# Second token mixing of a fused mixer network: the order of token splits, middle-layer splits and residuals on the vector and scalar engines

## The reference, cut to what matters

```python
def _moe2_ref(x, w_tok1, w_tok2, w_ch1, w_ch2):
    xt = x.transpose(0, 2, 1)
    h = np.maximum(xt @ w_tok1, 0.0) @ w_tok2      # 576 tokens -> 256 -> 576 tokens
    u = x + h.transpose(0, 2, 1)
    h2 = np.maximum(u @ w_ch1, 0.0) @ w_ch2        # 512 channels -> 1536 -> 512
    return (u + h2).astype(np.float32)
```

## Time and profile before

| | |
|---|---|
| time, median of 3 runs | 1283.67 us (1279.82 to 1286.72) |
| time of the profiled execution | 1284.21 us |
| its span in the profile | 1282.4 us |
| PE busy | 1206.6 us (94% of the span) |
| DVE busy | 820.4 us (64%) |
| ACT busy | 502.9 us (39%) |
| POOL busy | 368.4 us (29%) |
| granted TensorE clock, mean | 0.973 |

### The profile page before, as it was taken

How to read it: one execution, slowest core, us unless ns; L and a number is a source line. 1 busy time by engine, 2 the same in 40 slices (tenths; PEclk the granted TensorE clock), 3 DMA queues, 4 the chain that set the end, 5 groups by cost and what they waited for, 6 DMA issues and landing times.

```text
span 1282.4 us, 20593 instructions
## 1 busy us (share of the span) xinstructions
PE 1206.6 (94%) x7590; PEld 1168.7 (91%) x7590; DVE 820.4 (64%) x1220; ACT 502.9 (39%) x796; POOL 368.4 (29%) x216
## 2 busy tenths in 40 slices
PE   5989999999999999988687999999999899999998
PEld 5889999999898999887576899999999899999998
DVE  3776776676767676755353547667666775666664
ACT  3533334252425243423312245555555543333331
POOL 3443425344444424320641122322221420000000
PEclk9999999999999999989888999999999999999999
DMA  9824444352717230508737487867659999999982
GB/s 254 160 44 100 75 106 78 87 97 53 131 37 145 39 74 0 151 4 254 251 128 271 157 295 261 275 245 267 228 222 313 343 358 274 258 278 269 278 207 50
DMA packets 348428, 228.12 MB, mean 178 GB/s; under 512 B 268880, under 2 KB 316368, under 8 KB 347344
## 3 DMA queue, kind: packets, MB, share of 16 engines
q1 hardware_dynamic: 348368, 227.32, 61.6%
HBM read 136.84 MB, written 92.80 MB: 179 GB/s over the span
## 4 chain that ended last, share of the span: by engine, by line
PE 59%; issue 13%; DVE 10%; DMA 8%; POOL 4%; SPq 3%; ACT 2%; DVEq 0%; POOLq 0%; ACTq 0%
PE bank L42 11%; PE bank L43 10%; PE bank L44 10%; PE bank L1193 8%; PE bank L1194 8%; PE bank L1195 8%; DMA qkv_x_tokens<-x_tokens_scratch 3%; PE bank L252 2%; DVE weights_fraction L621 1%; SPq L154 1%; POOL z_z L797 1%; DVE tokens_cos L618 1%; DMA weights_down<-w_scratch 1%; DMA tokens_down<-w_scratch 1%; DVE attention_u L1094 1%
## 5 line engine op out<-in xcount | busy, mean ns | idle before, releaser
L42 PE MATMUL bank<-weights_tok,z_z 128*128 128x288 f32 x576 | 175.5, 305 | 14.7 <-ACT z_z L471 9.2
L43 PE MATMUL bank<-weights_tok,z_z 128*128 128x288 f32 x576 | 171.3, 297 | 0.0
L44 PE MATMUL bank<-weights_tok,z_z 128*128 128x288 f32 x576 | 171.2, 297 | 0.0
L42 PEld LDWEIGHTS bank<-weights_tok,z_z 128*128 128x128 f32 x576 | 109.8, 191 | 18.2 <-ACT z_z L471 10.6
L43 PEld LDWEIGHTS bank<-weights_tok,z_z 128*128 128x128 f32 x576 | 109.8, 191 | 0.0
L44 PEld LDWEIGHTS bank<-weights_tok,z_z 128*128 128x128 f32 x576 | 109.6, 190 | 0.0
L782 POOL TENSOR_TENSOR weights_rms_inverse<-weights_mean_squares,weights_minus_half 128x8 f32<-128x8 f32 x40 | 65.5, 1637 | 139.2 <-DVE weights_mean_squares L588 139.1
L797 POOL TENSOR_TENSOR z_z<-tokens_cos,z_z 128x512 fp32r<-128x512 f32 x32 | 51.3, 1604 | 178.9 <-ACT z_z L471 178.1
L478 ACT ACTIVATE weights_x_channel_major<-attention_u 128x288 fp32r<-128x288 f32 x64 | 28.4, 444 | 151.5 <-DVE attention_u L650 151.5
L42 PE MATMUL bank<-weights_x_channel_major,weights_ch 128*128 128x288 f32 x256 | 77.2, 301 | 0.0
L43 PE MATMUL bank<-weights_x_channel_major,weights_ch 128*128 128x288 f32 x256 | 75.4, 294 | 0.0
(11 more groups left out here) (272 smaller groups left out, 3750.8 us busy)
## 6 DMA issues: line engine op xcount, KB each, us to landing
g_scratch<-attention_staged SPq DMA_DIRECT2D x36, 960.0 KB, 4.6
weights_g<-g_scratch SPq DMA_DIRECT2D x24, 1152.0 KB, 8.3
g_scratch<-attention_staged SPq DMA_DIRECT2D x36, 384.0 KB, 4.7
x_scratch<-attention_u SPq DMA_DIRECT2D x8, 1152.0 KB, 4.5
u_scratch<-attention_u SPq DMA_DIRECT2D x8, 1152.0 KB, 9.9
weights_raw_u<-u_scratch SPq DMA_DIRECT2D x6, 1536.0 KB, 8.2
qkv_u_left<-u_scratch SPq DMA_DIRECT2D x12, 768.0 KB, 9.7
qkv_k<-in_k_dram SPq DMA_DIRECT2D x32, 256.0 KB, 5.0
```

Of the source, the lines that this page charges most:

```text
L42: eng.matmul(out, w[0], x[0], start=first, stop=False)
L43: eng.matmul(out, w[0], x[1], start=False, stop=False)
L44: return eng.matmul(out, w[1], x[0], start=False, stop=last)
```

## The change

Two orders are changed, and no instruction is added or taken away.

- ACT, for each batch: before, the first token piece of the next batch, then both halves of the middle layer, then the other token pieces. After: the middle layer's first half, the first token piece, the middle layer's second half, then the other token pieces.
- DVE, for each batch: before, both low parts of the middle layer, then the three token pieces of the next batch ahead of residuals 0, 2 and 4. After: first low part, first token piece, second low part, the other two token pieces, and then all eight residuals.

```diff
@@ phase_b, scalar
         def batch(n):
+            hidden_hi(n, 0)
             if n + 1 < B:
                 x_hi(act, n + 1, 0)
-            for mt in range(NM):
-                hidden_hi(n, mt)
+            hidden_hi(n, 1)
             for piece in range(1, NPX):
                 if n + 1 < B:
                     x_hi(act, n + 1, piece)
@@ phase_b, vector
         def batch(n, i, pair, more=True):
-            for mt in range(NM):
-                hidden_lo(n, mt)
+            hidden_lo(n, 0)
+            if more:
+                x_lo(dve, n + 1, 0)
+            hidden_lo(n, 1)
+            for piece in range(1, NPX):
+                if more:
+                    x_lo(dve, n + 1, piece)
             for g in range(NG):
-                if more and g % 2 == 0 and g // 2 < NPX:
-                    x_lo(dve, n + 1, g // 2)
                 residual(n, i, pair, g)
                 if isinstance(pair, int) and (n, g) in PREP_LO:
                     nxt["prep_lo"](dve, 0, PREP_LO[n, g])
```

## The result

The changed kernel takes 1254.28 us (median of 4 runs, 1252.93 to 1255.22) against 1283.75 (median of 4 runs) for the kernel before: a ratio of 0.9771 with a 95% interval of 0.9743 to 0.9799. The forecast was 1253. A second set of five runs gave 1252.43 us (0.9762, 0.974 to 0.9783). The profiled execution took 1252.93 us with a span of 1251.1.

The account below looks back on a forecast made before the run. PE was taken to stall because the middle layer queued on ACT behind the next token load. Gains of 33.7 us less losses of 2.9 gave 30.8, so 1284.2 became 1253.4, forecast 1253; own range 1249 to 1259, overall 1248 to 1270.

Parts of the forecast that it names:

- The cycle and its bound: Middle layer of batch n queues on ACT behind batch n + 1's token load; bound by PE, a batch takes 12.8 us.
- Part 1, ACT's order: On ACT, the first middle-layer half no longer waits for the token load; weight step done by E + 3.6.
- Part 2, DVE's order: On DVE, second low part by E + 1.65, 0.75 us before PE needs it; token pieces done by E + 3.4.
- E: The end of hidden(n), the hidden matmuls of batch n on PE; the forecast's times count from it.
- Part 3, what moves with it: SP issues the token load at E + 3.4, with nearly 2 us of room; the store just fits before residual 0.
- The sum: Over PE's mixes: 23.2 us of stalls plus 9.8 of half clock, 33.0; with batch 1's 0.7, 33.7 us.
- Batch 1: PE's mt 1 begins at 621.1, idling 4.9 us instead of 5.61, clock low as before: +0.7 us gain.
- (a): In batch 1 POOL may get in ahead of DVE's small token piece, delaying group 6; bounds 0 and 1.5, 0.7 us taken.
- (b): Batches 5 and 6: late store 4 and line 1249's load delay residuals; bounds 0 and 5, 2.2 us taken.
- POOL's lock in every batch: Rival, 0.08: POOL wins over DVE's small token piece in batches 1 to 4, costing 16 us in all: 1268.
- Load still late: Rival, 0.17: token load takes 9.6 us, cycle 14.3 us, PE idle between mt 0 and mt 1: 1270, or 1261.

Follow-up runs that it names:

- the half clock alone: Kernel before, with 32 extra matmuls of 288 columns on PE filling the stall ahead of each mix of batches 1 to 6: 1280.18 us (0.9973).
- the pieces in a row: Kernel before, with all three token pieces on DVE behind both low parts and ahead of residual 0, ACT as before: 1271.4 us (0.9894).
- one residual ahead: Changed kernel, with residual 0 of each batch moved ahead of the second and third token pieces on DVE: 1278.52 us (0.9962).
- with POOL only writing: Pieces in a row, with POOL's channel-weight work replaced by clearing, so it reads nothing and output is not the reference's: 1255.18 us (0.9781).

## Why the prediction was right

*The cycle and its bound.* Right. The load's wait is gone, and a batch bound by PE takes 12.75 us where 12.8 was worked out. The clock is 1.00 in batches 2 to 4, and ACT's wait for the load fell from 72.0 to 4.3 us.

*Part 1, ACT's order.* I described it as what frees the middle layer. It does so mainly in batch 1, where the first half of the mix runs during the wait. In the others the load is there in time, and the old order costs little: PE waits 0.81 us for ACT in batch 3, and the time is 1256.08 us against 1254.28, which the intervals do not tell apart. That the two parts are not alike in weight the prediction did not say.

*Part 2, DVE's order.* The times were right (the last piece done at E + 3.8 instead of 3.4, second low part well before it is needed). What was not seen is that the old order tied the load to the store, by way of residual 0, and to POOL. The prediction gave DVE's order the load's earlier issue; it did not say that ACT's order alone would fail, and the expectation for that run missed by 9 us for the same reason.

*Part 3, what moves with it.* Right, and narrowly: residual 0 waits 0.28, 0.18 and 0.70 us for the store in three batches, the load lands before it is wanted, and with its issue 4.3 to 6.0 us later nearly the whole gain is lost.

*The sum.* 33.7 us for stalls and half clock, of which 29.5 were measured between batch 1 and batch 7, after the losses. As a count of what PE would no longer lose it held. As two separate gains it did not: the half clock alone, mended in four batches, gave 0.4 us from batch 1 to 7. That the time came within 1 us of the forecast is in part luck: the two profiled executions of the changed kernel took 87.5 and 90.8 us from batch 1 to 7, with 0.2 us between their times.

*Batch 1.* Forecast +0.7 less 0.7 for POOL, measured -0.2. PE idles 4.77 us in the middle of the mix and then 1.48 ahead of group 6, which is (a) at its upper bound: POOL, which had asked meanwhile, got in between two DVE pieces. The rows of the changed kernel, DVE and POOL:

```profile
617.56 2.24 DVE L1068 TENSOR_TENSOR tokens_x_token_major<-qkv_x_tokens,tokens_x_token_major 128x1024 fp32r<-128x1024 f32 x1 [4.64 <-ACT tokens_x_token_major L1019]
...
621.57 3.85 DVE L1071 TENSOR_TENSOR tokens_x_token_major<-qkv_x_tokens,tokens_x_token_major 64x512 fp32r<-64x512 f32 x1
```

```profile
620.93 3.94 POOL L1145 TENSOR_TENSOR weights_up<-weights_raw_up,weights_up 128x1536 fp32r<-128x1536 f32 x1 [2.21 <-ACT weights_up L1040]
```

*The loss (b) in batches 5 and 6.* The size was near by luck (2.2 forecast, 2.6 + 0.3 measured), as the cause was wrong. In batch 5 residual 0 did not wait for store 4, and the load of line 1249 held DVE for 0.1 us at most. ACT stood still before the small token piece, the small low piece and residual 0 behind it, and PE behind that (ACT, DVE and PE of the changed kernel):

```profile
677.64 0.63 ACT L1019 ACTIVATE tokens_x_token_major<-qkv_x_tokens 128x512 fp32r<-128x512 f32 x1 [3.56 <-issue]
```

```profile
678.30 0.69 DVE L1071 TENSOR_TENSOR tokens_x_token_major<-qkv_x_tokens,tokens_x_token_major 64x512 fp32r<-64x512 f32 x1 [2.96 <-ACT tokens_x_token_major L1019]
```

```profile
679.53 0.40 PE L42 MATMUL bank<-qkv_tok,z_hidden_tok 128*128 128x288 f32 x1 [2.31 <-DVE attention_u L1094]
```

ACT waited for nothing that the profile shows; before, the same instruction had 1.98 us of this, hidden. ACT stands still ahead of this one instruction in every profile taken here, for 1.98 to 3.75 us. In both kernels it falls in a stretch with the DMA engines full (share 1.03 and 1.04), and instruction transfers lie around it. That code loading stands behind the data is thus argued, not shown; it was not tried. The 0.3 us of batch 6 follow from the same: the residuals of batch 5 were late, so was their store, and residual 0 of batch 6 waited 0.70 us for it. Only this last step is as (b) had it.

*The rivals.* "POOL's lock in every batch" had 0.08 and did not come, but only by 0.68 us. The runs with the pieces in a row (1271) and with one residual ahead (1278) are that rival, at the price worked out for it (1268) and above. Its chance should perhaps have been larger: with the vector engine's order alone the distance fell to 0.06 us in batch 3, though in both profiles of the changed kernel it was 0.68 in batches 2 to 4. "Load still late" did not come; it needed the load 4.3 to 6.0 us later.

The Trainium skill, SBUF — State Buffer, section "Who interferes with whom", has the rule that a VectorE instruction with two SBUF inputs excludes a GpSimd instruction that reads SBUF, and not one that only writes. The runs agree: with reads, line 1071 takes 3.9 us at the median in the kernel with the pieces in a row; with POOL only writing, 0.69 at the median and 0.693 at most, though in batch 2 POOL's clearing (637.27 to 638.66) lies over the whole of DVE's piece (637.39 to 638.08).

## What to carry to other kernels

Before a wait is removed, follow the loop that comes next in length, through single buffers (here a store that gates a residual) and in-order queues: taking the visible wait away on ScalarE alone gave 8 us of 30. Where VectorE and GpSimd hold each other up as here, what matters of VectorE's order is which instruction starts before GpSimd asks; under 0.8 us more or less decided 15 us here, so look for the next start on GpSimd beside each VectorE operation with two SBUF inputs, and count how much room there is. A step that frees the next load belongs ahead of work that can be late without harm.

## What the runs showed of the hardware

- When POOL asks while one DVE subtraction with two SBUF inputs runs and another of the same kind follows at once, POOL goes in between: the second one took 3.85, 3.82 and 3.91 us in three kernels instead of 0.69. A row of such operations on DVE is no protection. One that had started 0.06 us ahead of POOL was not held (0.69).
- The granted clock behind a short stall is not the same each time. In the profiled execution of the changed kernel the matmuls behind the stall of 2.31 us in batch 5 ran at 1.00; in another execution of the same kernel, with a stall there of 2.49 us, the next 4 us had 0.63, and a stall of 0.74 us in batch 1, which followed others, was followed by 0.58 (columns as in the earlier trace rows). From batch 1 to 2 it took 22.97 us and from 5 to 6 16.83, against 20.80 and 15.34.

```profile
679.50:683.00 3.50, 3.47 (x20) 3.17 (x21) 3.37 (x8) 0.85 (x1) 0.90 (x1) 1.00 0.75 244
```

```profile
679.40:683.40 4.00, 3.97 (x17) 3.79 (x18) 3.56 (x8) 0.84 (x1) 1.55 (x1) 0.63 0.77 253
...
623.90:628.50 4.60, 4.54 (x17) 4.27 (x18) 2.74 (x8) 0.00 (x0) 4.60 (x2) 0.58 0.86 274
```
